# Attention and two mixtures of experts: batched transfers in the front, a softmax sum from ScalarE's accumulator, and GpSimd converting a second weight

## The reference

```python
def _attn_ref(x, inducing):            # x: 2 x 11456 x 128, inducing: 32 x 128
    scale = 1.0 / np.sqrt(C)
    def mab(q, kv):
        s = scale * (q @ kv.transpose(0, 2, 1))
        s = s - s.max(-1, keepdims=True)
        a = np.exp(s)
        a /= a.sum(-1, keepdims=True) + 1e-09
        return a @ kv
    h = mab(I, x)                      # 32 inducing points look at all points
    return mab(x, h)                   # every point looks at the 32
...
x = _moe_ref(x, expert_emb, tau, w1, w2)                         # 8 experts, 128 -> 1024 -> 128
x = _moe2_ref(x, modality_id, w_gate, modality_bias, w1, w2)     # 8 experts, 128 -> 1024 -> 128
```

## Time and profile before

| what | value |
|---|---|
| median of 3 runs | 1131.33 us (1130.93 to 1133.27) |
| the profiled execution | 1135.07 us, its span 1133.3 us |
| mean granted TensorE clock | 0.95 of 2.4 GHz |
| TensorE, VectorE, ScalarE, GpSimd busy | 88%, 67%, 61%, 18% of the span |
| chain that ended last | PE 81%, SPq 6%, DMA 5% |
| bytes moved by the DMA engines | 64.70 MB |

### The profile page before, as it was taken

The page is one execution under the profiler, slowest core; times in us unless marked ns, Lnnn a source line. Parts: engine busy times, 40 slices in busy tenths (PEclk is TensorE's granted clock), DMA queues, the critical chain, the costliest instruction groups (busy, mean ns, idle before and its releaser), DMA issues.

```text
span 1133.3 us, 28294 instructions
## 1 busy us (share of the span) xinstructions
PE 1001.1 (88%) x6551; PEld 510.2 (45%) x6551; DVE 758.2 (67%) x2211; ACT 686.4 (61%) x1656; POOL 198.7 (18%) x438
## 2 busy tenths in 40 slices
PE   5266446589999999999999999999999999999886
PEld 4144312245445454555455554454554545554342
DVE  3144457566767777777777686767677777777563
ACT  3134346356666676666666666666666766666453
POOL 2691000211111111111111111111111111111000
PEclk9688769699999999999999999999999999999998
DMA  4976665000110101010000010001001010100000
GB/s 129 275 225 218 215 215 172 22 20 28 27 28 19 36 19 32 23 29 26 27 27 27 27 27 27 27 27 27 27 19 35 18 33 22 29 25 20 21 11 20
DMA packets 68615, 64.70 MB, mean 57 GB/s; under 512 B 9570, under 2 KB 60770, under 8 KB 68568
## 3 DMA queue, kind: packets, MB, share of 16 engines
q1 hardware_dynamic: 68568, 64.11, 19.0%
HBM read 40.55 MB, written 23.55 MB: 57 GB/s over the span
## 4 chain that ended last, share of the span: by engine, by line
PE 81%; SPq 6%; DMA 5%; issue 3%; DVE 2%; ACT 2%; POOL 1%; ACTq 0%; DVEq 0%; POOLq 0%
PE y L1224 42%; PE up L1247 22%; PE up L1237 7%; DMA stage<-in_moe_w 2%; SPq L301 2%; DMA GW<-in_x 2%; PE y L1311 2%; SPq L303 2%; PE up L1163 1%; PE TB L1271 1%; PE SM L1295 1%; SPq L316 1%; PE SM L1283 1%; SPq L310 1%; PE TB L1259 1%
## 5 line engine op out<-in xcount | busy, mean ns | idle before, releaser
L811 DVE SCALAR_TENSOR_TENSOR hlo<-up,hhi 128x500 f16<-128x500 f32 x736 | 490.2, 672 | 205.5 <-ACT hhi L560 203.0
L560 ACT ACTIVATE hhi<-up 128x500 f16<-128x500 f32 x736 | 415.5, 586 | 143.3 <-PE up L1237 75.9
L1247 PE MATMUL up<-ytb,W1B 128*128 (+1 forms) x1104 | 277.7, 382 | 17.4 <-issue 14.8
L1224 PE MATMUL y<-hhi,W2A 128*128 128x500 f16 x736 | 217.1, 376 | 1.1 <-DVE hlo L811 1.1
L1224 PE MATMUL y<-hhi,GW 128*128 128x500 f16 x736 | 216.0, 374 | 0.5 <-DVE hlo L811 0.4
L1247 PEld LDWEIGHTS up<-ytb,W1B 128*128 x1104 | 108.6, 99 | 155.8 <-issue 48.2
L1237 PE MATMUL up<-E4T,GW 128*128 (+1 forms) x368 | 138.4, 380 | 0.0
L1224 PE MATMUL y<-hlo,W2A 128*128 128x500 f16 x368 | 137.8, 374 | 0.0
L1224 PE MATMUL y<-hlo,GW 128*128 128x500 f16 x368 | 137.6, 374 | 0.0
L476 POOL TENSOR_TENSOR st<-ss,root 125x4 f32<-125x4 f32 x46 | 46.8, 1018 | 374.5 <-ACT TB L592 374.5
L1224 PEld LDWEIGHTS y<-hhi,W2A 128*128 x736 | 67.8, 97 | 66.6 <-issue 15.5
(11 more groups left out here) (158 smaller groups left out, 1053.5 us busy)
## 6 DMA issues: line engine op xcount, KB each, us to landing
x_turned<-GW SPq DMA_DIRECT2D x46, 250.0 KB, 4.1
xth<-x_turned SPq DMA_DIRECT2D x46, 250.0 KB, 2.6
out<-yout SPq DMA_DIRECT2D x46, 250.0 KB
GW<-in_x SPq DMA_DIRECT2D x46, 240.0 KB
stage<-in_moe_w SPq DMA_DIRECT2D x16, 512.0 KB, 4.2
W1B<-in_moe_w SPq DMA_DIRECT2D x8, 512.0 KB, 7.2
w2s<-in_moe_w SPq DMA_DIRECT2D x8, 512.0 KB, 3.9
GW<-in_x SPq DMA_DIRECT2D x46, 10.0 KB
```

Source lines behind the costliest of these rows:

```text
L560: nc.scalar.activation(hhi[:, (u % UP) * CT:(u % UP + 1) * CT], ups[u % UP][:, 0:CT], ACT.Relu).then_inc(s["hi_done"], 1)
L811: nc.vector.scalar_tensor_tensor(hlo[:, o:o + CT], ups[u % UP][:, 0:CT], 0.0, hhi[:, o:o + CT], ALU.max, ALU.subtract).then_inc(s["lo_done ...
L1224: ins = mm(y[:, 0:CT], W[:, bass.ds(woff + (fb * 2 * C + o), C)], h[:, k * CT:(k + 1) * CT], start=opens and fb == 0 and n == 0, stop=fb = ...
L1247: ins = mm(ups[k][:, 0:CT], W1B[:, bass.ds(woff + (wl * F + fb * P), P)], ytb[:, bass.ds(yoff + yl * CW, CT)], start=n == 0, stop=n == 2)
```

## The change

- x is loaded by two transfers for a whole quad, 120 and 5 partitions, in runs of 2,048 B (the appended column is gone), and a quad is stored by one transfer. All three wait for, and signal, whole quads.
- The softmax sum comes from ScalarE's accumulator in `exp_points`. A new VectorE step, `keep_twice`, copies out the weights of the two points that the next chunk has again, and they are subtracted at the end. The per-quad sums are weighted by a new `share`.
- SP starts with quad 0 of x, before the constants. The weights are spread: `w2a` 0 and 1 between the first quads, then one weight after each quad's load, `w2a` 2 to 7 and then `w1b` 0 to 5, the last two after the loop.
- GpSimd converts `w1b` too, after `w2a`, with the same three instructions, from a ring of four slots (`stage` and `w2s` together). The first `w1a` loads wait for `w1b` conversions 5 and 6, the first two `w2b` loads for 7 and 8.
- TensorE starts when the identity and the inducing points are there, and no longer after GpSimd's whole setup. The expert embeddings' squares move behind quad 0 on VectorE.

```diff
+            def load_points(q):
+                gs, slot, whole = CHUNKS[q], q % XR_N, TQ // 8 * 8
+                for p0, p1 in ((0, whole), (whole, TQ)):
+                    r0 = row0(sp, gs[0]) + p0 * TJ
+                    points = bass.AP(xf.tensor, r0 * C, [[TJ * C, p1 - p0], [STEP * C, len(gs)], [1, TJ * C]])
+                    sp.dma_start(xr[p0:p1, slot, 0:len(gs), :], points).then_inc(s[f"x_loaded{slot}"], 16)
+
+            def load_w1b(e):
+                if e >= 4:
+                    sp.wait_ge(s["w1b_steps"], 3 * (e - 3))
+                sp.dma_start(wraw[:, e % 4, :], w1b[e, :, :]).then_inc(s[f"w1b_loaded{e % 4}"], 16)
+
+            load_points(0)
+            sp.dma_start(ind[:, :], inducing).then_inc(s["inducing_loaded"], 16)
+            load_points(1)
+            load_w2a(0)
...
+            load_points(2)
+            load_w2a(1)
+            load_points(3)
             for q in range(NQ):
...
+                gs = CHUNKS[q]
+                sp.wait_ge(s["lo_ready"], gs[-1] + 1)
+                sp.dma_start(XTD[gs[0]:gs[-1] + 1, :, :].rearrange("g p n -> p g n"),
+                             xT[:, q % XT_N * STREAMS:q % XT_N * STREAMS + len(gs), :]).then_inc(
+                    s[f"x_stored{q % XT_N}"], 16)
                 if q >= 1 and q - 1 + XR_N < NQ:
                     sp.wait_ge(s["mixed_in"], q)
                     load_points(q - 1 + XR_N)
+                if q + 2 < NE:
+                    load_w2a(q + 2)
+                elif q + 2 < 2 * NE:
+                    load_w1b(q + 2 - NE)
+            for e in range(NQ + 2 - NE, NE):
+                load_w1b(e)
...
                 if e < 2:
-                    sp.wait_ge(s["w_lo_ready"], NE - 1 + e)
+                    sp.wait_ge(s["w1b_steps"], 3 * (e + 5))
...
-                if e >= 2:
+                if e < 2:
+                    sp.wait_ge(s["w1b_steps"], 3 * (e + 7))
+                else:
                     sp.wait_ge(s["w2b_lo_ready"], e - 1)
...
+            for e in range(NE):
+                raw = wraw[:, e % 4, :]
+                hi, lo, a = high_low(gp, "w1", W1B, e, raw)
+                gp.wait_ge(s[f"w1b_loaded{e % 4}"], 16 * (e // 4 + 1))
+                nc.gpsimd.tensor_scalar(raw, raw, S_W, None, ALU.mult).then_inc(s["w1b_steps"], 1)
+                gp.wait_ge(s["w1b_steps"], 3 * e + 1)
+                nc.gpsimd.tensor_copy(hi, a).then_inc(s["w1b_steps"], 1)
+                gp.wait_ge(s["w1b_steps"], 3 * e + 2)
+                nc.gpsimd.tensor_tensor(lo, a, hi, ALU.subtract).then_inc(s["w1b_steps"], 1)
...
                 nc.scalar.activation(pex[:, q % 2, :], sbank(q)[:, 0:CT], ACT.Exp, bias=bias[:, q:q + 1],
-                                     scale=SCALE_I).then_inc(s["exp_ready"], 1)
+                                     scale=SCALE_I, accum_out=sums[:, q:q + 1]).then_inc(s["exp_ready"], 1)
...
+            def keep_twice(q):
+                v.wait_ge(s["exp_ready"], q + 1)
+                once = M * (len(CHUNKS[q]) - (q % QB == QB - 1))
+                if once < P:
+                    nc.vector.memset(twice[:, q, :], 0.0).then_inc(s["twice_clear"], 1)
+                    v.wait_ge(s["twice_clear"], q // QB + 1)
+                nc.vector.tensor_copy(twice[0:once, q, :],
+                                      pex[0:once, q % 2, CT - TQ * (CT - STEP - 1) - 1:CT:TQ]).then_inc(
+                    s["twice_kept"], 1)
...
+                keep_twice(q)
+                if q == 0:
+                    expert_squares()
+                    v.wait_ge(s["pool_setup"], 1)
...
+            for k in range(CT - STEP):
+                link(nc.vector.tensor_tensor(sums[:, :], sums[:, :], twice[:, :, k], ALU.subtract))
...
+            link(nc.vector.tensor_tensor(sums[:, :], sums[:, :], share[:, :], ALU.mult))
             for b in range(NB):
-                link(nc.vector.tensor_scalar(hw[:, b, :], hacc[:, b, :], mw[:, b:b + 1], None, ALU.mult))
+                link(nc.vector.tensor_reduce(hw[:, b, C:C + 1], sums[:, b * QB:(b + 1) * QB], X, ALU.add))
+                link(nc.vector.tensor_scalar(hw[:, b, 0:C], hacc[:, b, 0:C], share[:, (b + 1) * QB - 1:(b + 1) * QB],
+                                             None, ALU.mult))
...
-            pe.wait_ge(s["pool_setup"], 1)
-            pe.wait_ge(s["consts_loaded"], 16 * 5)
+            pe.wait_ge(s["ident_ready"], 1)
+            pe.wait_ge(s["inducing_loaded"], 16)
...
-                        ins = mm(y2[k * M:(k + 1) * M, 0:C + 1], pexT[0:rows, q % 2, j * P + k * M:j * P + (k + 1) * M],
-                                 xr[0:rows, q % XR_N, k, j, :], start=j == 0, stop=j == TJ - 1)
+                        ins = mm(y2[k * M:(k + 1) * M, 0:C], pexT[0:rows, q % 2, j * P + k * M:j * P + (k + 1) * M],
+                                 xr[0:rows, q % XR_N, k, j * C:(j + 1) * C], start=j == 0, stop=j == TJ - 1)
```

More of the change, by code:

```diff
@@ L98, in attention_two_moe_kernel @@
         xto = sb("xto", [P, 2, CT], f16)[:, :, :]
-        stage = sb("stage", [P, 2, F])
-        w2s = sb("w2s", [P, 2, F])
+        wraw = sb("wraw", [P, 4, F])
+        stage, w2s = wraw[:, 0:2, :], wraw[:, 2:4, :]
         xth = sb("xth", [P, 2 * CT + 4], f16)
@@ L112, in attention_two_moe_kernel @@
         alpha = sb("alpha", [P, NQ])
+        sums = sb("sums", [P, NQ])
+        twice = sb("twice", [P, NQ, CT - STEP])
+        share = sb("share", [P, NQ])
         sel4 = sb("sel4", [P, M])
@@ L285, in _, with as_w2, load_w2a @@
         def _(sp):
-            for dst, src in ((ind[:, :], inducing), (en[:, :], expert_emb), (wg[:, :], w_gate)):
+            def as_w2(slot):
+                return slot.rearrange("p (f c) -> p f c", c=C)
+            def load_points(q):
[4 more added lines that the diff above has]
+                    sp.dma_start(xr[p0:p1, slot, 0:len(gs), :], points).then_inc(s[f"x_loaded{slot}"], 16)
+            def load_w2a(e):
+                sp.dma_start(as_w2(w2raw[:, e, :]), w2a[e, :, :].rearrange("(f p) c -> p f c", p=P)).then_inc(
+                    s[f"w2a_loaded{e // 2}"], 16)
+            def load_w1b(e):
[6 more added lines that the diff above has]
+            load_w2a(0)
+            for dst, src in ((en[:, :], expert_emb), (wg[:, :], w_gate)):
                 sp.dma_start(dst, src).then_inc(s["consts_loaded"], 16)
@@ L319, in _ @@
                     load_points(q - 1 + XR_N)
-            for e in range(NE):
-                if e >= 2:
[L322 to L326, removed]
+                if q + 2 < NE:
[4 more added lines that the diff above has]
+                load_w1b(e)
+            for slot in range(XT_N):
+                sp.wait_ge(s[f"x_stored{slot}"], 16 * len(range(slot, NQ, XT_N)))
             def load(q):
@@ L525, in _ @@
             for b in range(NB):
[L526 to L532 removed]
+                nc.scalar.activation(share[:, b * QB:(b + 1) * QB], bias[:, b * QB:(b + 1) * QB], ACT.Exp,
+                                     bias=mneg[:, b:b + 1], scale=-1.0).then_inc(s["weights_ready"], 1)
             for k in range(NB + 4 * NE):
@@ L1079, in turn_points @@
                 q, k = quad_of(g)
-                pe.wait_ge(s[f"x_loaded{q % XR_N * STREAMS + k}"], 32 * (earlier(q, k, XR_N) + 1))
+                pe.wait_ge(s[f"x_loaded{q % XR_N}"], 32 * (q // XR_N + 1))
                 if g >= 3:
```

113 lines of the change are left out of this document (42 added, 71 removed).

## The result

The changed kernel takes 1115.8 us (median of 4 runs, 1112.48 to 1116.97) against 1131.3 us; the ratio is 0.9847, 95% interval 0.9819 to 0.9876. It is faster, clear of the noise, but by 15.5 us (1.5%) and not by the 40 us forecast, and it lies above the range of 1083 to 1109 us. The profiled executions differ by more than the medians, 22.6 us: that of after (1112.48 us) was the fastest of its runs, that of before was 3.7 us above its median. So the profiles show about 7 us more gain than the medians do.

A forecast was written before the change was run, and what follows sets the result against it. SP's issue was taken to bound the front, then DMA, with GpSimd's weight conversions next. The main loop would start at 151.6 us, 40.0 us sooner; 1131.3 - 40.0 gave 1091 us, range 1083 to 1109 us.

The forecast's parts named there:

- the pace of a quad: Front: DMA engines become the bound at 7.2 us a quad, between 5.2 us (TensorE) and 8.8 us (today's pace).
- The start: Before the front: TensorE waits only for the inducing points, turns the first chunk 3.1 us sooner; first scores at 14.7 us.
- rival 1: Front stays at SP's or DMA's old pace, 8.8 us a quad; main loop at 169 us, 1109 us; chance 0.18.
- Issue: SP's queue in the front: cost is per transfer, merged ones cost no more, so issue falls to 2.5 us a quad.
- The end of the front: Last scores to the products: 11.7 us as before plus 1.8 us of added VectorE work, 13.5 us; products from 107.4 us.
- Rival 2: Front and its end: VectorE waits for GpSimd's current instruction, pace 8.0 us, end 11 us longer; 1100 us, chance 0.12.
- GpSimd: Weight conversion, the next bound: sixteen at 6.08 us, 97.3 us, from 20.7 us, with 2.5 us waiting, ending at 120.5 us.
- The products: Between front and main loop: expert 2 at 125.1 us, then 26.5 us to the main loop at 151.6 us.
- The stall of 20.1 us: TensorE's wait before the change for `w1a` behind the `w1b` conversion; forecast gone, with a shorter one in its place.

The follow-up runs named there:

- e1_x128: Changed kernel with each quad of x (except the last) loaded by one transfer of 128 partitions instead of two of 120 and 5: 1094.1 us.
- e3_chunks: Changed kernel with x loaded by eight unpadded transfers a quad (120 and 5 partitions for every chunk) instead of two: 1104.8 us.
- e8_gp0: Changed kernel, loads of 120 and 5 partitions kept, with ScalarE and VectorE converting all eight `w1b` behind the front instead of GpSimd: 1109.4 us.
- e12_gp0_x128: Kernel with 128-partition loads, with ScalarE and VectorE converting all eight `w1b` behind the front instead of GpSimd: 1085.5 us.

## Why the prediction was wrong

**The step that failed** is in the part on the pace of a quad: "The DMA engines need 2.05 MB at 371 GB/s, 5.5 us", and from it 7.2 us a quad. The 371 GB/s came from stores of 128 partitions and was used for loads of 120 and 5. For those no row could tell: in the earlier trace rows x alone moved 152 GB/s at a share of 0.53, which is 287 GB/s at a full share, but such a division says nothing about what happens when the queue is full. Measured were 200 GB/s with x nearly alone and 294 GB/s in the settled front, and 8.2 us a quad. With 128 partitions (e1_x128) the same two rates are 327 and 371 to 373 GB/s, and the kernel comes within 2.8 us of the forecast: 1094.1 against 1091.3 us. That the DMA engines become the bound, and GpSimd behind them, was right; the price of x in them was not.

**Step by step.**

- *The start.* Forecast: first scores at 14.7 us. They came at 18.20 us, because the inducing points stood behind 1.02 MB that moved at 200 instead of 371 GB/s. With 128 partitions: 15.2 us.
- *The pace.* Forecast 7.2 us; it was (108.14 - 18.20) / 11 = 8.2 us, and 6.3 us with 128 partitions. The prediction had named a pace over 8 us as what would be wrong, and gave paces of 7.7 to 8.8 us 0.18, as rival 1. That rival is what came, with its loop at 169 us against 170.85 us measured, though for neither of its two reasons: a merged issue costs 0.32 us when nothing holds it up, and the DMA engines' share is full.
- *Issue.* The prediction read "the cost is per transfer" from the 0.76 us of the small load. The number of transfers was not what made it dear: unpadded loads of the same size cost 0.29 us at least and 0.36 us at the median (e3_chunks). It did no harm to the sum, but it credited the wrong part of the change.
- *The end of the front.* Forecast 13.5 us from the last scores; it was 124.88 - 108.14 = 16.7 us. Rival 2, VectorE waiting for GpSimd, happened beside the forecast and not in its place: `mT4b` took 1.72 us against 0.21 us before, and the copies of the kept weights spread widely (view of that line, minimum, median, maximum ns):

```profile
L711 DVE COPY twice<-pex x12: 158/704/1984, 22.8 to 111.7; 128x2 f32<-128x2 f32 x10, 64x2 f32<-64x2 f32 x2
```

  The rule of the Trainium skill (SBUF — State Buffer, section "SBUF: two separate sides") agrees with this trace. The 1.72 us of `mT4b` end 0.1 us after the GpSimd instruction beside them (113.89 to 116.02 us), and without `w1b` on GpSimd the same copy takes 0.22 us. But the wait can be longer than the one instruction that the prediction took as its limit: 4.58 us, through three of them, in the kernel with four `w1b` on GpSimd. At the end of the front it cost 4.1 us here (16.2 against 12.1 us in e8_gp0, start to start), 4.7 us with 128 partitions (e12_gp0_x128), and not the 11 us of the rival.
- *GpSimd.* The 6.08 us a weight held, and so did the order of the bounds. Its start was 5.4 us late (26.1 for 20.7 us), and it waited 19.1 us where 2.5 us stood, 2.1 us of them before the first weight. The end was 140.2 us for 120.5 us. This is where the rate hit hardest: a pair of `w2a` comes with two quads, each 8.2 us long. The prediction had one place for a slow pace, rival 1, and took the lateness of `w1b` 5 there, not of `w2a`. Its 1109 us were too low an end for a second reason: the 40 us were a difference to one profiled execution that stood 3.7 us above its median, and were taken from the median. By the profiled executions the change gained 22.6 us, by the medians 15.5 us.
- *The products.* Expert 2 at 145.6 for 125.1 us, 5.4 us behind GpSimd's end (4.6 forecast), and from there 25.2 us to the loop (26.5). These terms held, and so did the length of the main loop (939.9 for 942 us).

**Where the missing time went.** Of the 40.0 us forecast 20.7 us came, by loop starts. The missing 19.3 us are the loads of 120 and 5 partitions, 19.9 us (170.85 against 151.00 us); with 128 partitions the loop starts 0.6 us sooner than forecast. By medians 24.5 us are missing: 21.7 us and 2.8 us. Part of that agreement is luck: with 128 partitions the pace was 6.3 us for 7.2 and the end of the front 17.3 us for 13.5, errors of opposite sign, and both lay hidden behind GpSimd's chain. Of what was gained, the GpSimd part of the change gave nothing: without it the changed kernel is faster (1109.4 us). The stall of 20.1 us is 7.7 us at most in the changed kernel, but only 10.6 us also without `w1b` on GpSimd (e8_gp0); so most of it went with the rest of the change, and that it was the earlier loads of `w1b` is argued, not shown. Dropping the padded column, which the forecast gave no price of its own, was worth 20 us with eight loads a quad, and merging them took 11 us of that back.

**What stays open.** Why x, loaded over 120 and 5 partitions, comes at about 0.6 of the rate (200 against 327 GB/s), with packets that take twice as long. The Trainium skill (DMA: Bandwidth & Descriptors, section "Why a DMA increments its semaphore by 16 and not by 1") says that a transfer uses the largest number of engines up to 16 that divides the slowest dimension on both of its sides: 15 for 120, 16 for 112 and 128. By that page one engine missing of 16 would cost 6% (an estimate), and 112 partitions were slow too, so this rule alone does not explain it. That the engines meet at the same doors of SBUF is argued, not shown. That the small second transfer of 5 or 13 partitions has a part in it is not ruled out: every slow form has one, and only the fast form has none. Why merged loads over 120 partitions were 11 us slower than eight is open too; the rate from 2 to 10 us was 200 GB/s against 251. No run undoes ScalarE's accumulator and `keep_twice`, or TensorE's earlier start, by themselves.

## What to carry to other kernels

A rate read from one kind of transfer is no price for another: the shape over the partitions belongs to the rate, as bytes and runs do, and a view with the DMA engines at a share of 0.5 doesn't show the rate at 1.0. Before transfers are merged, look at why their issue is dear; here a padded row of 129 numbers was the reason, and one load of 128 partitions with three rows too many, instead of two of 120 and 5, was worth 22 us. When work is moved to an idle engine, compute when that engine ends and not how idle it is, and whom it slows on the way: half of the `w1b` on GpSimd was 11 us better than all; over none its lead of 2 us is not clear of the noise.

## What the runs showed of the hardware

- Loads of x in runs of 2,048 B, DMA share about 1.0, from 2 to 10 us: 128 partitions 327 GB/s, 120 and 5 partitions 200 GB/s merged and 251 GB/s in eight transfers, 112 and 13 partitions 250 GB/s. A packet of x took 84, 162, 107 and 121 ns in them (medians, in the same order). With another step in HBM (2,304 B) and 120 partitions 203 GB/s from 10 to 20 us.
- SP's issue of a load, eight a quad: 0.85 us in runs of 512 B with a step of 129 numbers in SBUF, 0.36 us in runs of 2,048 B (medians), 0.73 and 0.29 us at least. Merged, two a quad, in the changed kernel: 0.32 us at least, 1.51 us at the median, up to 4.05 us.
- A VectorE copy of 128 x 2 numbers from SBUF to SBUF: 0.16 us at least, up to 1.98 us while GpSimd converts weights (the changed kernel), and 3.53 us through the end of a conversion and two memsets of GpSimd (e12_gp0_x128).
